# Fused attention and feed-forward kernel: the last tokens of each head projected on quarter tiles, and the weight product in one piece between the projections

## The chip, the cores and the metric

One core of one Trainium2 chip. The metric is the device time of one execution in microseconds, lower is better. Before the change, the median of three runs is 926.65 us (926.5 to 930.34).

## The reference

```python
def phi(x):                                  # x: (4, 8, 576, 64), w_phi: (64, 128)
    proj = np.einsum('bhsd,df->bhsf', x, w_phi)
    proj = proj - np.max(np.abs(proj), axis=-1, keepdims=True)
    return np.concatenate([np.exp(proj), np.exp(-proj)], axis=-1)
q_p, k_p = phi(q), phi(k)
kv = np.einsum('bhsf,bhsd->bhfd', k_p, v)
z = np.sum(k_p, axis=2)
num = np.einsum('bhsf,bhfd->bhsd', q_p, kv)
den = np.einsum('bhsf,bhf->bhs', q_p, z)[..., None] + 1e-06
x = (num / den) -> (2304 tokens, 512)
h = ((x @ w1) * (x @ w2)) @ w3               # w1, w2: 512x1024, w3: 1024x1024
x = h @ w_out                                # 1024x512
r = np.maximum(x @ w_in, 0.0)                # 512x2048
out = (r * r) @ w_out2                       # 2048x512
```

All arrays are float32.

## The kernel before

The kernel has two stages on one core. The first is attention over 16 pairs of heads, to about 253 us of the span. It also makes the product w3 @ w_out, so that the first feed-forward needs one matrix where the reference has two. The second stage is both feed-forwards; the change doesn't touch it.

Each engine has its instruction stream written out by hand, and the streams meet on semaphores; nothing reorders them. A pair is two heads of 576 tokens, one in partitions 0 to 63 (h0), the other in 64 to 127 (h1), features by tokens. 576 tokens are four chunks of 128 and a tail of 64. One pair on TensorE, in order:

1. `first_half`: wait for k's load, for the previous zq and for the previous tail exponential; project k (`project`, L459 the chunks, L461 the tail) into `ps_proj`; the numerators of the previous pair's first half of tokens (L482, with 64-column tiles, and L490, the denominators with 32-column tiles); a quarter of a weight product (L551, six matmuls); wait for q and for zk; project q; the numerators of the second half of tokens.
2. `second_half`: `kv_sign(0)` (L466, L468), another quarter of the weight product, wait for zq, `transpose_features` (L474, L475), `kv_sign(1)`.

The quarters of the weight product run from pair 3 on: 24 matmuls for each of eight 128-row pieces of w3, of which pairs 3 to 15 do two quarters each; the last three halves come after the pairs. In a projection the tokens are the stationary operand. Each chunk is a 64-row matmul, alternating between the row halves; the tail is one 128-row matmul over both heads, whose operand is padded: the two heads' tails stand in separate columns with zeros in the other head's rows, so q and k have 640 columns instead of 576, and phi is stored in three blocks. A float32 matmul is two load and two matmul instructions in the trace.

DVE, per pair: after the k projection a reduction to the largest absolute value (L588) and an addition (L593) give zk; then a piece of the previous output (L280); the same for q gives zq; then the low halves of the weight product (L610) and of the next w3 piece (L86); the inverse of the denominators (L272, L274). ACT: copies of numerators (L667), exponentials of zk (L660), the high halves of the weight product (L693) and of w3 (L80), exponentials of the transposed zq (L648 for the tail, L652), a copy of kv (L673). SyncE issues all transfers in one hand-written order; the loads of q, k and v for a pair go out about one pair ahead. DVE and ACT split the first unit of feed-forward weights behind pair 3 as well (L186, L180).

Of the kernel before, what the change touches and what calls it, by code (L numbers as in the profile page):

```python
# [23 lines left out]
P = 128  # L24
BATCH, HEADS, SEQ, HEAD_DIM, FEAT = 4, 8, 576, 64, 128
PAIRS = BATCH * HEADS // 2
# [2 lines left out]
CHUNKS = SEQ // P  # L29
TAIL = SEQ - CHUNKS * P  # L30
FULL = CHUNKS * P
WIDE = FULL + 2 * TAIL
SLOTS = 2 * CHUNKS + 1
VW = HEAD_DIM + 1

# [253 lines left out]
def attention(nc, ins, ident_dram, x_dram, d_dram, r_dram, wprod, raw, ff):  # L289
    qT, kT, v_full, v_tail, w_phi, wout_dram, w3_dram, wu_dram = ins  # L290
    with ExitStack() as ctx:  # L291
        def sb(name, shape, dt=F32):
            return ctx.enter_context(nc.sbuf_tensor(name, shape, dt))
# [6 lines left out]

        ident = sb("ident", [P, P])

        phi_raw = sb("phi_raw", [P, 3, FEAT])
        q_raw = [sb(f"q_raw{s}", [P, WIDE]) for s in range(2)]
        k_raw = [sb(f"k_raw{s}", [P, WIDE]) for s in range(2)]
        vs = [sb(f"vs{s}", [P, CHUNKS + 1, 2, VW]) for s in range(2)]
        neg_max_k = sb("neg_max_k", [P, SLOTS])
        neg_max_q = sb("neg_max_q", [P, SLOTS])
# [46 lines left out]
        @block.sync  # L355
        def _(sp):
            def load_qkv(n, s, reused):

                if reused:
                    sp.wait_ge(kproj_done, n - 1)  # L360
                sp.dma_start(k_raw[s][:, :], kT[n]).then_inc(k_loaded[s], 16)
                if reused:
                    sp.wait_ge(qproj_done, n - 1)
                sp.dma_start(q_raw[s][:, :], qT[n]).then_inc(q_loaded[s], 16)
                if reused:
                    sp.wait_ge(kv_done, n - 1)
                load_v(n, s)

            def load_v(n, s):
                for h in range(2):  # L370
                    sp.dma_start(vs[s][:, 0:CHUNKS, h, 0:HEAD_DIM], v_full[n, :, :, h]).then_inc(v_loaded[s], 16)
                sp.dma_start(vs[s][:, CHUNKS, :, 0:HEAD_DIM], v_tail[n]).then_inc(v_loaded[s], 16)

            sp.dma_start(k_raw[0][:, :], kT[0]).then_inc(k_loaded[0], 16)
            sp.dma_start(phi_raw[:, :, :], w_phi).then_inc(phi_loaded, 16)
            sp.dma_start(q_raw[0][:, :], qT[0]).then_inc(q_loaded[0], 16)
            sp.dma_start(ident[:, :], ident_dram).then_inc(ident_loaded, 16)

            sp.wait_ge(v_framed, 2)
            load_v(0, 0)  # L380
            load_qkv(1, 1, False)
            for i in range(2):
                sp.dma_start(raw.slots[i][:, :], wout_dram[i]).then_inc(raw.loaded[i], 16)

            def load_piece(slot, src, pieces):

                sp.wait_ge(raw.lo, pieces)
                sp.dma_start(raw.slots[slot][:, :], src).then_inc(raw.loaded[slot], 16)

            def results(n, s):  # L390

                store_den(sp, ff, n - 1, 1 - s, 1, d_dram)
                load_den(sp, ff, n - 1, d_dram)
                spread_rden(sp, ff, n - 1, r_dram)

            for i in range(2, WOUT_CHUNKS):
                load_piece(i % 2, wout_dram[i], i - 1)
            store_den(sp, ff, 0, 0, 0, d_dram)
            load_qkv(2, 0, True)
            results(1, 1)  # L400
            load_piece(0, w3_dram[0], WOUT_CHUNKS - 1)
            sp.wait_ge(raw.lo, WOUT_CHUNKS)
            load_unit(sp, ff, wu_dram, 0)
            store_den(sp, ff, 1, 1, 0, d_dram)
            load_qkv(3, 1, True)
            store_x(sp, ff, 0, x_dram)
            results(2, 0)
            store_den(sp, ff, 2, 0, 0, d_dram)
            load_qkv(4, 0, True)
            load_piece(0, w3_dram[1], PIECE_W3 + 1)  # L410
            store_x(sp, ff, 1, x_dram)
            results(3, 1)


            with sp.Fori(2, PAIRS // 2 - 1) as i:
                store_den(sp, ff, 2 * i - 1, 1, 0, d_dram)
                load_qkv(2 * i + 1, 1, True)
                store_x(sp, ff, 2 * i - 2, x_dram)
                results(2 * i, 0)
                store_den(sp, ff, 2 * i, 0, 0, d_dram)  # L420
                load_piece(0, w3_dram[i], PIECE_W3 + i)
                load_qkv(2 * i + 2, 0, True)
                store_x(sp, ff, 2 * i - 1, x_dram)
                results(2 * i + 1, 1)
            store_den(sp, ff, PAIRS - 3, 1, 0, d_dram)
            load_qkv(PAIRS - 1, 1, True)
            store_x(sp, ff, PAIRS - 4, x_dram)
            results(PAIRS - 2, 0)
            store_den(sp, ff, PAIRS - 2, 0, 0, d_dram)
            load_piece(0, w3_dram[KF1 - 1], PIECE_W3 + KF1 - 1)  # L430
            load_x(sp, ff, x_dram, 0)
            store_x(sp, ff, PAIRS - 3, x_dram)
            results(PAIRS - 1, 1)
            sp.wait_ge(raw.lo, PIECE_W3 + KF1)
            load_unit(sp, ff, wu_dram, 1)
            store_den(sp, ff, PAIRS - 1, 1, 0, d_dram)
            store_x(sp, ff, PAIRS - 2, x_dram)
            store_den(sp, ff, PAIRS - 1, 1, 1, d_dram)
            load_den(sp, ff, PAIRS - 1, d_dram)
# [13 lines left out]
        def _(pe):  # L453
            def project(src):

                for c in range(CHUNKS):
                    for h in range(2):
                        rows = slice(h * HEAD_DIM, (h + 1) * HEAD_DIM)
                        pe.matmul(ps_proj[:, CHUNKS * h + c, :], src[rows, c * P:(c + 1) * P], phi_raw[rows, h, :],  # L459
                                  start=(c == 0), stop=True, skip_group_check=True)  # L460
                return pe.matmul(ps_proj[:, 2 * CHUNKS, :], src[:, FULL:WIDE], phi_raw[:, 2, :], start=True, stop=True)  # L461

            def kv_sign(sign, s):
                for h in range(2):
# [31 lines left out]
            def first_half(n, s, turn, w=None):  # L496


                pe.wait_ge(k_loaded[s], 16 * (turn + 1))
                pe.wait_ge(zq_done, n)  # L500
                pe.wait_ge(eq_tail_done, n)
                project(k_raw[s]).then_inc(kproj_done, 1)
                if previous(n):
                    first_numerators(n - 1)
                if w:
                    w_product(*w)

                pe.wait_ge(q_loaded[s], 16 * (turn + 1))
                pe.wait_ge(zk_done, n + 1)
                project(q_raw[s]).then_inc(qproj_done, 1)  # L510
                if previous(n):
                    last_numerators(n - 1)
# [8 lines left out]
                pe.wait_ge(ff.num_copied, 2 * n + 1)  # L521
                numerators(1).then_inc(numB_done, 1)

            def second_half(n, s, turn, w=None):

                pe.wait_ge(v_loaded[s], 48 * (turn + 1))
                pe.wait_ge(ek_done, 2 * n + 1)

                pe.wait_ge(kv_copied, n)
                kv_sign(0, s)  # L530
                if w:
                    w_product(*w)

                pe.wait_ge(zq_done, n + 1)
                pe.wait_ge(eq_done, n)
                transpose_features().then_inc(t_done, 1)
                pe.wait_ge(ek_done, 2 * n + 2)
                kv_sign(1, s).then_inc(kv_done, 1)

            def w_product(m, part, parts=4):  # L540

                if part == 0:

                    pe.wait_ge(raw.hi, m + PIECE_W3 + 1)
                    pe.wait_ge(wp_lo, m)
                steps = [(i, a, b, k) for i, (a, b) in enumerate(TERMS) for k in range(KF1)]
                n = len(steps) // parts
                for i, a, b, k in steps[part * n:(part + 1) * n]:
                    if a == LO and k == 0:
                        pe.wait_ge(raw.lo, m + PIECE_W3 + 1)  # L550
                    last = pe.matmul(ps_w[:, :], w3[:, a, k * P:(k + 1) * P],  # L551
                                     wout[:, b, k * D_MODEL:(k + 1) * D_MODEL],
                                     start=(i == 0 and k == 0), stop=(i == 2 and k == KF1 - 1))
                if part == parts - 1:
                    last.then_inc(wp_done, 1)

            pe.wait_ge(phi_loaded, 16)
# [6 lines left out]
            first_half(2, 0, 1)  # L564
            second_half(2, 0, 1)
            first_half(3, 1, 1, (0, 0))
            second_half(3, 1, 1, (0, 1))
            with pe.Fori(2, PAIRS // 2) as i:
                first_half(2 * i, 0, i, (i - 2, 2))
                second_half(2 * i, 0, i, (i - 2, 3))  # L570
                first_half(2 * i + 1, 1, i, (i - 1, 0))
                second_half(2 * i + 1, 1, i, (i - 1, 1))

            w_product(KF1 - 2, 1, 2)
            first_numerators(PAIRS - 1)
            w_product(KF1 - 1, 0, 2)
            last_numerators(PAIRS - 1)
            w_product(KF1 - 1, 1, 2)


        @block.vector
# [612 lines left out]
```

## Time and profile before

| | before |
|---|---|
| median of three runs | 926.65 us |
| lowest, highest | 926.5, 930.34 us |
| profiled execution, its own time | 926.82 us |
| its span | 925.0 us |
| TensorE matmul, load | 900.7 us (97%), 796.7 us (86%) |
| DVE, ACT, GpSimd | 584.9 us (63%), 409.3 us (44%), 219.4 us (24%) |
| mean granted TensorE clock | 0.998 of full speed |

Busy times are shares of the span. PE is TensorE's matmul side, PEld its weight loads, which run beside matmuls. In an operand shape such as 64\*128 the first number is the rows that a tile of the array uses and the second its columns. The ends of matmuls are modelled and overlap the next ones, so it is starts that should be compared.

### The profile page before, as it was taken

To read this page: it belongs to the slowest core of one execution; us is meant where nothing else is said; L and a number is where in the kernel's file an instruction comes from. 1 tells how busy PE (TensorE), PEld (TensorE's weight loads), DVE (VectorE), ACT (ScalarE), POOL (GpSimd) and SP (SyncE) were. 2 spreads that over 40 slices of the span, in tenths; PEclk is the share of its full clock that TensorE was granted. 3 is DMA by queue.
4 is the path that set the end of the run, shared out by engine and by line. 5 is a ranking of instruction groups with operands and counts; after the bars stand their busy time and mean duration, and the time that the engine had idled before them with its cause. 6 is when DMAs were issued, how large, how long until landed. Compare 5 with 4: busy or idle time off the path is not lost. (4 is left out here: it accounts for less than half of the span.)

```text
span 925.0 us, 15179 instructions
## 1 busy us (share of the span) xinstructions
PE 900.7 (97%) x5712; PEld 796.7 (86%) x5712; DVE 584.9 (63%) x732; ACT 409.3 (44%) x675; POOL 219.4 (24%) x222
## 2 busy tenths in 40 slices
PE   6889999999989999999999999999999999999998
PEld 6768787777679999999999998989889888989897
DVE  3554545454467666666666678776777776666652
ACT  3534543444443445344534464444544344634433
POOL 0100000000336324432353216322143222213100
PEclk9999999999999999999999999999999999999999
DMA  6544345352441112311331232321133212132201
GB/s 188 158 117 138 100 129 147 109 154 83 153 162 35 52 44 102 115 46 46 114 114 46 69 136 86 121 90 48 62 144 114 92 46 91 46 119 87 69 23 69
DMA packets 62023, 89.32 MB, mean 97 GB/s; under 512 B 29840, under 2 KB 40464, under 8 KB 61200
## 3 DMA queue, kind: packets, MB, share of 16 engines
q1 hardware_dynamic: 61968, 88.58, 29.3%
q8 instruction: 35, 0.57, 0.3%
q14 instruction: 20, 0.16, 0.1%
HBM read 74.26 MB, written 14.30 MB: 96 GB/s over the span
## 5 line engine op out<-in xcount | busy, mean ns | idle before, releaser
L851 PE MATMUL banks<-xc,wc 128*128 128x384 f32 x2016 | 411.3, 339 | 7.7 <-PEq L291 3.5
L851 PEld LDWEIGHTS banks<-xc,wc 128*128 128x128 f32 x2016 | 360.2, 189 | 31.5 <-issue 6.6
L931 ACT COPY s<-banks 128x384 f32<-128x384 f32 x144 | 69.1, 480 | 236.7 <-PE banks L851 236.7
L155 POOL TENSOR_TENSOR w_raw<-w_raw 128x256 f32<-128x256 f32 x48 | 37.3, 778 | 442.5 <-DMA w_raw<-in_w_units 442.5
L1042 DVE TENSOR_TENSOR c<-s,banks 128x384 f32<-128x384 f32 x144 | 79.5, 552 | 95.1 <-PE banks L851 60.7
L186 DVE TENSOR_TENSOR wc<-w_raw,wc 128x1024 fp32r<-128x1024 f32 x96 | 117.9, 1236 | 23.9 <-ACT wc L180 23.9
L1051 DVE TENSOR_TENSOR pg<-c,pg 128x384 fp32r<-128x384 f32 x120 | 93.9, 788 | 44.2 <-ACT pg L938 43.4
L895 PE MATMUL banks<-wprod_hi,pg 128*128 128x512 f32 x432 | 113.0, 393 | 0.0
L895 PE MATMUL banks<-wprod_lo,pg 128*128 128x512 f32 x432 | 112.2, 393 | 0.0
L938 ACT CAST pg<-c 128x384 fp32r<-128x384 f32 x120 | 61.9, 515 | 93.9 <-DVE c L1099 55.4
L873 PE MATMUL banks<-pg,wprod_hi 128*128 128x256 f32 (+1 forms) x384 | 97.8, 338 | 1.0 <-DVE pg L1051 1.0
L895 PEld LDWEIGHTS banks<-wprod_lo,pg 128*128 128x128 f32 x432 | 80.0, 188 | 12.2
L180 ACT CAST wc<-w_raw 128x1024 fp32r<-128x1024 f32 x96 | 90.5, 945 | 0.0
L895 PEld LDWEIGHTS banks<-wprod_hi,pg 128*128 128x128 f32 x432 | 80.0, 188 | 11.9
L873 PEld LDWEIGHTS banks<-pg,wprod_hi 128*128 128x128 f32 x384 | 68.0, 188 | 1.9 <-DVE pg L1051 1.9
L873 PE MATMUL banks<-pg,wprod_lo 128*128 128x512 f32 x192 | 65.2, 340 | 0.0
L466 PEld LDWEIGHTS ps_kv<-vs,ek 128*128 128x128 f32 x512 | 61.3, 196 | 3.4 <-issue 3.4
L466 PE MATMUL ps_kv<-vs,ek 128*128 128x65 f32 x512 | 63.9, 279 | 0.0
L201 POOL TENSOR_TENSOR x_sum<-x_raw 128x768 f32<-128x768 f32 x6 | 12.4, 2065 | 193.5 <-DMA x_raw<-x_raw_dram 193.5
L551 PE MATMUL ps_w<-wout,w 128*128 128x512 f32 x192 | 51.9, 408 | 0.0
L160 POOL TENSOR_TENSOR w_raw<-w_raw 128x256 f32<-128x256 f32 x48 | 48.9, 1020 | 0.0
L1046 DVE SCALAR_TENSOR_TENSOR c<-c 128x384 f32<-128x384 f32 x72 | 46.9, 652 | 2.5
(68 smaller groups left out, 930.5 us busy)
## 6 DMA issues: line engine op xcount, KB each, us to landing
w_raw<-in_w_units SPq DMA_DIRECT2D x48, 384.0 KB, 3.9
wo_raw<-in_w_out SPq DMA_DIRECT2D x24, 512.0 KB, 3.5
w_raw<-in_w_units SPq DMA_DIRECT2D x48, 128.0 KB, 3.9
k_raw<-in_kT SPq DMA_DIRECT2D x16, 320.0 KB, 3.0
q_raw<-in_qT SPq DMA_DIRECT2D x16, 320.0 KB, 3.9
stage<-r_dram SPq DMA_DIRECT2D x32, 144.0 KB, 3.0
x_raw_dram<-stage SPq DMA_DIRECT2D x16, 288.0 KB, 3.5
x_raw<-x_raw_dram SPq DMA_DIRECT2D x3, 1536.0 KB, 6.6
```

What stands on the lines that cost most here:

```text
L160: pool.tensor_tensor(s4, a12, s2, ALU.subtract).then_inc(ff.s4_made, 1)
L180: act.copy(hi, raw).then_inc(ff.wc_hi, 1)
L186: dve.tensor_tensor(lo, raw, hi.bitcast(F32), ALU.subtract).then_inc(ff.wc_lo, 1)
L466: pe.matmul(ps_kv_v[:, sign, h, :], ek[:, sign, CHUNKS * h + c, :], vs[s][:, c, h, :], start=(c == 0 and h == 0 and sign == 0), stop=False ...
L551: last = pe.matmul(ps_w[:, :], w3[:, a, k * P:(k + 1) * P], wout[:, b, k * D_MODEL:(k + 1) * D_MODEL], start=(i == 0 and k == 0), stop=(i ...
L851: last = pe.matmul(bank, ff.wc[u % 2][:, w, i, k * P:(k + 1) * P], x[:, a, k, :], start=(i in (P1, P2, P5) and t == 0 and k == 0), stop=(t ...
L873: last = pe.matmul(acc[b][:, cols], wprod[w][:, j * D_MODEL + n * P:j * D_MODEL + (n + 1) * P], pg[u % 2][:, a, 0, tokens], start=(j == 0 ...
L895: last = pe.matmul(acc[c], pg[u % 2][:, a, f, c * P:(c + 1) * P], wo[u % 2][:, w, f * D_MODEL:(f + 1) * D_MODEL], start=(j == 0 and m == 0 ...
L931: act.copy(out[:, :], y_bank).then_inc(copied, 1)
L938: act.copy(pg[u % 2][:, HI, f, half * TB:(half + 1) * TB], raw[:, :]).then_inc(pg_hi, 1)
L1042: dve.tensor_tensor(out[:, :], {P2: s1, P5: s3, P3: s2}[i][:, :], z_bank, ALU.add).then_inc(done, 1)
L1051: dve.tensor_tensor(pg[u % 2][:, LO, f, cols], raw[:, :], pg[u % 2][:, HI, f, cols].bitcast(F32), ALU.subtract).then_inc(pg_lo, 1)
```

## The change

The tail of each head becomes a matmul of its own, with 64 rows and 64 stationary columns (64 tokens), in the head's row half and with its output in the head's partition half. The order is h0 chunk 0, h1 tail, h0 chunk 1, h1 chunk 0, h0 chunk 2, h1 chunk 1, h0 chunk 3, h1 chunk 2, h0 tail, h1 chunk 3. The weight product runs in halves of twelve matmuls, all between the two projections, and none in `second_half`. q and k lose their padding (576 columns), phi is 128 by 128 and is the first transfer.

```diff
-        phi_raw = sb("phi_raw", [P, 3, FEAT])
-        q_raw = [sb(f"q_raw{s}", [P, WIDE]) for s in range(2)]
-        k_raw = [sb(f"k_raw{s}", [P, WIDE]) for s in range(2)]
+        phi_raw = sb("phi_raw", [P, FEAT])
+        q_raw = [sb(f"q_raw{s}", [P, SEQ]) for s in range(2)]
+        k_raw = [sb(f"k_raw{s}", [P, SEQ]) for s in range(2)]
...
+            sp.dma_start(phi_raw[:, :], w_phi).then_inc(phi_loaded, 16)
             sp.dma_start(k_raw[0][:, :], kT[0]).then_inc(k_loaded[0], 16)
-            sp.dma_start(phi_raw[:, :, :], w_phi).then_inc(phi_loaded, 16)
             sp.dma_start(q_raw[0][:, :], qT[0]).then_inc(q_loaded[0], 16)
...
             def project(src):
 
-                for c in range(CHUNKS):
-                    for h in range(2):
-                        rows = slice(h * HEAD_DIM, (h + 1) * HEAD_DIM)
-                        pe.matmul(ps_proj[:, CHUNKS * h + c, :], src[rows, c * P:(c + 1) * P], phi_raw[rows, h, :],
-                                  start=(c == 0), stop=True, skip_group_check=True)
-                return pe.matmul(ps_proj[:, 2 * CHUNKS, :], src[:, FULL:WIDE], phi_raw[:, 2, :], start=True, stop=True)
+
+                def chunk(h, c):
+                    rows = slice(h * HEAD_DIM, (h + 1) * HEAD_DIM)
+                    if c < CHUNKS:
+                        return pe.matmul(ps_proj[:, CHUNKS * h + c, :], src[rows, c * P:(c + 1) * P],
+                                         phi_raw[rows, :], start=(c == 0), stop=True, skip_group_check=True)
+                    return pe.matmul(ps_proj[rows, 2 * CHUNKS, :], src[rows, FULL:SEQ], phi_raw[rows, :],
+                                     start=True, stop=True, skip_group_check=True)
+
+                for c in range(CHUNKS + 1):
+                    chunk(0, c)
+                    last = chunk(1, (c - 1) % (CHUNKS + 1))
+                return last
...
-            def second_half(n, s, turn, w=None):
+            def second_half(n, s, turn):
...
                 kv_sign(0, s)
-                if w:
-                    w_product(*w)
...
-            def w_product(m, part, parts=4):
+            def w_product(m, part):
...
-                n = len(steps) // parts
+                n = len(steps) // 2
...
             first_half(3, 1, 1, (0, 0))
-            second_half(3, 1, 1, (0, 1))
+            second_half(3, 1, 1)
             with pe.Fori(2, PAIRS // 2) as i:
-                first_half(2 * i, 0, i, (i - 2, 2))
-                second_half(2 * i, 0, i, (i - 2, 3))
+                first_half(2 * i, 0, i, (i - 2, 1))
+                second_half(2 * i, 0, i)
                 first_half(2 * i + 1, 1, i, (i - 1, 0))
-                second_half(2 * i + 1, 1, i, (i - 1, 1))
```

The rest of the diff drops the host's padding of q, k and phi and adapts the three calls of `w_product` behind the loop, which do the same as before.

## Rows read from the trace of the kernel before

**Rows 1.** The page: busy time of the engines; the chain by engine.

```profile
PE 900.7 (97%) x5712; PEld 796.7 (86%) x5712; DVE 584.9 (63%) x732; ACT 409.3 (44%) x675; POOL 219.4 (24%) x222
...
PE 48%; DVE 1%; ACT 0%; issue 0%; ACTq 0%
```

**Rows 2.** Windows, one pair: busy time (instructions) by engine, granted clock, DMA.

```profile
152.41:167.11 14.70, 14.70 (x143) 11.52 (x142) 8.12 (x8) 6.69 (x12) 0.00 (x0) 1.00 0.37 108
```

**Rows 3.** Waits up to 300 us: total us, times, longest.

```profile
PE ps_proj L459 <- DVE zk L593: 8.3, 5, 2.9
```

**Rows 4.** TensorE in order of time: start, us from first start to last end.

```profile
152.41 1.16 PE L459 MATMUL ps_proj<-phi_raw,k_raw 64*128 64x128 f32 x16
153.50 0.49 PE L461 MATMUL ps_proj<-phi_raw,k_raw 128*128 128x128 f32 x2
153.92 1.19 PE L482 MATMUL ps_num<-eq,kv 128*64 128x288 f32 x8
155.04 0.70 PE L490 MATMUL ps_num<-eq,kv 128*32 128x144 f32 x16
155.67 1.66 PE L551 MATMUL ps_w<-wout,w 128*128 128x512 f32 x6
157.26 1.16 PE L459 MATMUL ps_proj<-phi_raw,q_raw 64*128 64x128 f32 x16
...
162.35 0.44 PE L468 MATMUL ps_kv<-vs,ek 128*128 128x130 f32 x2
162.54 1.64 PE L551 MATMUL ps_w<-wout,w 128*128 128x512 f32 x6
164.02 1.04 PE L474 MATMUL ps_t<-ident,zq 128*128 128x128 f32 x8
```

**Rows 5.** Weight loads in order of time, the same pair.

```profile
152.41 0.97 PEld L459 LDWEIGHTS ps_proj<-phi_raw,k_raw 64*128 64x128 f32 x16
...
155.04 0.40 PEld L490 LDWEIGHTS ps_num<-eq,kv 128*32 128x32 f32 x16 [0.44 <-issue]
```

**Rows 6.** Instructions of lines 459 and 482: duration in ns, least, median, most.

```profile
L459 PEld LDWEIGHTS ps_proj<-phi_raw,k_raw x256: 182/188/330, 4.3 to 226.7; 64*128 64x128 f32 x128
L459 PE MATMUL ps_proj<-phi_raw,k_raw x256: 271/272/578, 4.3 to 226.8; 64*128 64x128 f32 x128
...
L482 PEld LDWEIGHTS ps_num<-eq,kv x152: 132/137/138, 100.0 to 232.8; 128*64 128x64 f32 x152
```

**Rows 7.** In order of time: the first projection, and DVE behind the second pair's.

```profile
4.25 2.08 PE L459 MATMUL ps_proj<-phi_raw,k_raw 64*128 64x128 f32 x16 [4.25 <-DMA phi_raw<-in_w_phi]
...
6.26 0.79 PE L461 MATMUL ps_proj<-phi_raw,k_raw 128*128 128x128 f32 x2
...
21.99 1.36 DVE L588 TENSOR_REDUCE neg_max_k<-ps_proj 128x9 f32<-128x1152 f32 x1 [4.14 <-PE ps_proj L461]
```

**Rows 8.** Windows, the first 20 us.

```profile
0.00:20.00 20.00, 12.81 (x79) 12.10 (x80) 7.95 (x12) 7.12 (x9) 1.42 (x6) 1.00 0.67 195
```

**Rows 9.** TensorE in order of time, pair 2.

```profile
29.98 0.44 PE L468 MATMUL ps_kv<-vs,ek 128*128 128x130 f32 x2
30.26 1.04 PE L474 MATMUL ps_t<-ident,zq 128*128 128x128 f32 x8
```

**Rows 10.** TensorE in order of time, behind the last pair.

```profile
240.41 2.98 PE L551 MATMUL ps_w<-wout,w 128*128 128x512 f32 x12
```

**Rows 11.** In order of time: DVE in pair 3, TensorE in pairs 3 and 4.

```profile
48.74 1.16 DVE L86 TENSOR_TENSOR w<-w_raw,w 128x1024 fp32r<-128x1024 f32 x1
...
52.71 1.16 PE L459 MATMUL ps_proj<-phi_raw,q_raw 64*128 64x128 f32 x16 [1.41 <-DVE zk L593]
...
69.08 1.16 PE L459 MATMUL ps_proj<-phi_raw,q_raw 64*128 64x128 f32 x16 [1.61 <-DVE zk L593]
```

**Rows 12.** DVE in order of time, the pair of rows 4.

```profile
160.27 1.36 DVE L593 TENSOR_TENSOR zq<-ps_proj,neg_max_q 128x1152 f32<-128x1152 f32 x1
```

**Rows 13.** Transfers: KB each, median us from issue to landing.

```profile
k_raw<-in_kT SPq DMA_DIRECT2D x16, 320.0 KB, 3.0
```

More of the change, by code:

```diff
@@ L31 @@
 FULL = CHUNKS * P
-WIDE = FULL + 2 * TAIL
 SLOTS = 2 * CHUNKS + 1
@@ L553, in w_product @@
                                      start=(i == 0 and k == 0), stop=(i == 2 and k == KF1 - 1))
-                if part == parts - 1:
+                if part == 1:
                     last.then_inc(wp_done, 1)
@@ L566, in _ @@
             first_half(3, 1, 1, (0, 0))
-            second_half(3, 1, 1, (0, 1))
+            second_half(3, 1, 1)
             with pe.Fori(2, PAIRS // 2) as i:
-                first_half(2 * i, 0, i, (i - 2, 2))
-                second_half(2 * i, 0, i, (i - 2, 3))
+                first_half(2 * i, 0, i, (i - 2, 1))
+                second_half(2 * i, 0, i)
                 first_half(2 * i + 1, 1, i, (i - 1, 0))
-                second_half(2 * i + 1, 1, i, (i - 1, 1))
-            w_product(KF1 - 2, 1, 2)
+                second_half(2 * i + 1, 1, i)
+            w_product(KF1 - 2, 1)
             first_numerators(PAIRS - 1)
-            w_product(KF1 - 1, 0, 2)
+            w_product(KF1 - 1, 0)
             last_numerators(PAIRS - 1)
-            w_product(KF1 - 1, 1, 2)
+            w_product(KF1 - 1, 1)
         @block.vector
@@ L1145, in stacked @@
     def stacked(a):
-        t = a.transpose(0, 1, 3, 2).reshape(PAIRS, 2, HEAD_DIM, SEQ)
-        wide = np.zeros((PAIRS, 2, HEAD_DIM, WIDE), a.dtype)
-        wide[..., :FULL] = t[..., :FULL]
-        for h in range(2):
-            wide[:, h, :, FULL + h * TAIL:FULL + (h + 1) * TAIL] = t[:, h, :, FULL:]
-        return wide.reshape(PAIRS, P, WIDE)
+        return pack(a.transpose(0, 1, 3, 2).reshape(PAIRS, P, SEQ))
     qT, kT = stacked(q), stacked(k)
@@ L1160 @@
     v_tail = v_tail.reshape(PAIRS, P, 2, HEAD_DIM)
-    phi_blocks = np.zeros((P, 3, FEAT), w_phi.dtype)
-    for h in range(2):
-        rows = slice(h * HEAD_DIM, (h + 1) * HEAD_DIM)
-        phi_blocks[rows, h] = w_phi
-        phi_blocks[rows, 2] = w_phi
+    phi_twice = pack(np.concatenate([w_phi, w_phi]))
     w3 = pack(moe_w3.T.reshape(KF1, P, KF1, P).transpose(2, 1, 0, 3).reshape(KF1, P, W_CHUNK))
@@ L1185 @@
     arrays = {
-        "qT": qT, "kT": kT, "v_full": v_full, "v_tail": v_tail, "w_phi": phi_blocks, "w3": w3, "w_out": w_out,
+        "qT": qT, "kT": kT, "v_full": v_full, "v_tail": v_tail, "w_phi": phi_twice, "w3": w3, "w_out": w_out,
         "w_units": w_units, "w_out2": w_out2, "identity": np.eye(P, dtype=np.float32),
```

## The prediction

> **What bounds the kernel now.** I read the page first. TensorE is busy for 97% of the span, and the chain that ended last stays on it [rows 1], so the question is what the change does to TensorE's queue, not to DVE, ACT or the transfers. Every line of the diff belongs to attention, which ends near 253 us. The windows show what a pair is there: 14.70 us, TensorE busy for all of it, and two more pairs in a row take the same [rows 2]. So in the steady part, what TensorE's instructions take is what the pair takes. There are 16 pairs.
>
> The waits name the exceptions [rows 3]: in attention five waits of a projection of q for the shifted k (zk), one in each of pairs 0 to 4, 8.3 us together.
>
> The view in order of time then shows how one group of matmuls follows another [rows 4]. Ends are modelled, so I set each start against the modelled end before it. Where the shape stays 128\*128, the next group starts 0.16 to 0.25 us before that end: 162.54 against 162.35 + 0.44 = 162.79, 164.02 against 164.18. Where the shape changes it is always 0.07: 153.50 against 152.41 + 1.16 = 153.57 (64\*128 to 128\*128), 153.92 against 153.99 (to 128\*64), 155.04 against 155.11 (to 128\*32), 155.67 against 155.74 (to 128\*128), 157.26 against 157.33 (to 64\*128). After a change the first load starts with the first matmul, and the load side had sat idle 0.44 us before 155.04 [rows 5]. So a change of tile shape empties the pipe and then exposes the first load. The change to 128\*32 tells most: its first tile (columns 0 to 31) shares no column with the last one before it (64 to 127), and it waits all the same.
>
> The Trainium skill has this as a rule (TensorEngine Tiling (Array Packing), Key Properties): changing the tiling mode, not just the tile, drains TensorE. The five changes above agree with it. It lists 64×128 and 64×64 as two configurations; no row of this trace has a 64\*64 tile.
>
> **The change, part by part.**
>
> *Tail on quarter tiles.* A projection is now 16 half-array instructions, 153.50 − 152.41 = 1.09 us, and 2 full ones, 153.92 − 153.50 = 0.42: 1.51 us [rows 4]. After the change it is 20: a 64\*128 chunk (2), the h1 tail 64\*64 (2), six 64\*128 chunks (12), the h0 tail (2), a chunk (2). Four changes of shape inside are new, and the one to the full tail goes. The trace doesn't show a 64\*64 tile, so I bound it.
>
> - All four cost what every change here costs: then a lone matmul of two instructions is like the full tail, load exposed, second load behind it, drain: 0.42 us. A tail loads 64 columns, 0.137 us against 0.188 [rows 6]: 0.37. The run of twelve is that of sixteen less four steps; a step is (0.97 − 0.19)/15 = 0.052 by loads [rows 5], (1.16 − 0.27)/15 = 0.059 by matmuls [rows 4, 6]; with 0.055, 1.09 − 0.22 = 0.87. Sum 0.42 + 0.37 + 0.87 + 0.37 + 0.42 = 2.45, +0.94. The full tail is the nearest row (as many instructions, as wide an operand, a change on both sides), and I take this value.
> - Cheapest drain: only a longer step. The last half matmul started at 152.41 + 1.16 − 0.27 = 153.30, the next group at 153.50: 0.20 for 0.055. A lone matmul: (0.49 − 0.27)/2 = 0.11, and 0.20, 0.31; the twelve 11 × 0.059 + 0.20 = 0.85. Sum 2.09, +0.58.
> - Dearest: 4 × 0.42 + 0.85 = 2.53, +1.02.
> - No drain: 1.09 + 4 × 0.055 = 1.31, −0.20.
>
> *Where it counts.* In pairs 5 to 15 TensorE never waits, so both projections count. In pairs 0 to 2 the wait for zk runs from the end of the projection of k, for which DVE had been idle (4.14 us in pair 1 [rows 7]): both count too. In the first pair instructions take about twice as long (16 in 6.26 − 4.25 = 2.01 us, the tail 0.79 − 0.07 = 0.72), at a granted clock of 1.00 [rows 7, 8]: 2 × 0.72 + 2 × 0.62 + 2.01 − 4 × 0.12 = 4.21 against 2.73, +1.48. Pairs 3 and 4 are below. So 2 × 1.48 + 13 × 2 × 0.94 = 27.4 us.
>
> *Weight product in one piece.* Its 192 instructions stay; in pairs 3 to 15 the six behind kv_sign(0) move between the projections. Taken away: last kv group to transposes 164.02 − 162.35 = 1.67 us [rows 4], 30.26 − 29.98 = 0.28 in a pair without them [rows 9]: 1.39. Added: twelve before a change of shape take 2.98 − 0.07 = 2.91 [rows 10], six 157.26 − 155.67 = 1.59 [rows 4]: 1.32. Eleven pairs × −0.07 = −0.8; with 0.2 of doubt at an end, −3 to +1.5.
>
> *Pairs 3 and 4.* Here the six more cover a wait of the q projection for zk, 1.41 and 1.61 us. zk was late because DVE was in a split (48.74 + 1.16 = 49.90 in pair 3) when the k projection had long ended [rows 11]. That split hangs on the pair before, so a k projection 0.94 later is swallowed too. q then starts later by 0.94 + 1.32 − 1.41 = 0.85 and 0.65 us; with the q projection +0.94 and the six gone −1.39 that is +0.4 and +0.2, +0.6 together. With no drain q starts when zk lets it, as now, and each pair gives −0.20 − 1.39 = −1.59.
>
> *What the six covered behind kv_sign(0).* The transposes could start at 162.35 + 0.28 = 162.63 [rows 4, 9]; zq is done at 160.27 + 1.36 = 161.63 [rows 12]: 1.0 us to spare. ACT's and DVE's halves of the product come earlier, ahead of the exponentials of q instead of among them. The next k projection needs the tail exponential, the numerators the copy of kv; both move with the transposes or ahead, and TensorE waited for neither: nothing gained. SyncE's next w3 piece waits for DVE's half, now earlier.
>
> *Unpadded q and k, smaller phi, phi first.* 288 KB for 320 a load; a load of k lands in 3.0 us [rows 13] and is issued almost a pair ahead: hidden. At the start TensorE waits until 4.25 us for phi [rows 7], issued second; now k is second. With 3.0 us to land for k too it is 0, between −0.5 and +0.3.
>
> **Sum.** Against the profiled execution, 926.82 us (span 925.0; 0.2 above the runs' median): 926.8 + 27.4 − 0.8 + 0.6 = 954 us, +2.9%. Its own ends: cheapest 926.8 + 14 × 1.16 − 0.8 (pairs 3 and 4) − 0.8 = 941; dearest 926.8 + 13 × 2.04 + 3.4 + 0.9 + 1.5 = 959.
>
> **Rivals.**
> *No drain (the other side).* The 64\*64 tiles flow within their row halves. For it: the halves overlap here, a step of 0.055 against 0.11 alone. Against: none of the five changes of shape escaped. It decides at each projection's second matmul: a start 0.05 after the first, not 0.4. 926.8 − 13 × 0.40 − 2 × 0.24 − 2 × 1.59 − 0.8 = 917 us.
> *Waiting within a row half only*, where a tail and a chunk follow each other in it: two waits of 0.15 (0.20 − 0.055), 1.31 + 0.30 = 1.61, +0.10. 14 × 0.20 + 2 × (0.10 − 1.39) − 0.8 = −0.6: 926 us. Against: the change to 128\*32, as above.
> *The transposes wait for zq*, from the point at which it is 1.0 us later; at most 1.39 × 13 = 18 us: with no drain, up to 935. Pair 2 has that order already, and its transposes follow the last kv group by only 0.28 [rows 9].
>
> **How the numbers follow.** Drain 0.70, no drain 0.17, within a half 0.11, zq 0.02. One measurement of this kernel tells 0.5% (4.6 us) from no change. Slower 0.70 + 0.02, same 0.11, faster 0.17. The likeliest alone: 941 to 959. The range takes in the within-a-half case and 4 us below it, and leaves out most of no drain: 921 to 960.
>
> **What would show it.** Right: matmuls of shape 64\*64 on TensorE, 64 each for k and q; a projection of about 2.45 us in order of time, each change of shape 0.07 before the modelled end; the load side idle inside it; a pair of 16.5 us; no wait for zk in pairs 3 and 4; everything behind attention shifted and otherwise alike. Wrong: 20 instructions in 1.3 us and a pair of 14.2; or a gap before the transposes put down to zq.

## The result, and the profile after

The changed kernel takes 956.07 us (median of four runs, 955.01 to 962.57); the kernel before, run on the same chip, 928.5 (926.5 to 930.61). The ratio on record is 1.031, 95% interval 1.026 to 1.037 (it is estimated from the runs, and is not exactly the quotient of the two medians, 1.030). The prediction was 954 us. The profiled execution after took 955.01 us, its span is 953.2, that is 28.2 more than before. One run of all that are told of here, 963.53 us in e6, stands as slow beside the others of its kernel, and its ratio leaves it out.

The page: TensorE's busy time has risen from 900.7 us [rows 1] by 32.1 us. That is 3.9 more than the span, because TensorE also waits less: 3.0 us for zk, 0.7 at the start of the feed-forward and 0.2 for the first load. DVE, ACT and GpSimd do what they did.

```profile
PE 932.8 (98%) x5776; PEld 812.9 (85%) x5776; DVE 584.5 (61%) x732; ACT 409.2 (43%) x675; POOL 220.9 (23%) x222
...
PE 47%; DVE 1%; ACT 0%; issue 0%; ACTq 0%
```

One steady pair in windows (busy time and instructions by engine, granted clock), to be read against [rows 2]: 16.47 us in place of 14.70, still with no idle TensorE, at a clock of 1.00 in both.

```profile
154.06:170.53 16.47, 16.47 (x146) 12.46 (x145) 6.49 (x7) 5.80 (x10) 0.00 (x0) 1.00 0.42 124
```

TensorE in order of time, the same stretch of a pair as [rows 4]. The lines that answer to them are the projections: what was two rows is five.

```profile
154.06 0.48 PE L459 MATMUL ps_proj<-phi_raw,k_raw 64*128 64x128 f32 x2
154.48 0.43 PE L461 MATMUL ps_proj<-phi_raw,k_raw 64*64 64x128 f32 x2
154.84 0.94 PE L459 MATMUL ps_proj<-phi_raw,k_raw 64*128 64x128 f32 x12
155.70 0.43 PE L461 MATMUL ps_proj<-phi_raw,k_raw 64*64 64x128 f32 x2
156.06 0.48 PE L459 MATMUL ps_proj<-phi_raw,k_raw 64*128 64x128 f32 x2
156.48 1.19 PE L488 MATMUL ps_num<-eq,kv 128*64 128x288 f32 x8
...
158.23 3.01 PE L555 MATMUL ps_w<-wout,w 128*128 128x512 f32 x12
161.17 0.49 PE L459 MATMUL ps_proj<-phi_raw,q_raw 64*128 64x128 f32 x2
...
167.17 0.44 PE L474 MATMUL ps_kv<-vs,ek 128*128 128x130 f32 x2
167.45 1.04 PE L480 MATMUL ps_t<-ident,zq 128*128 128x128 f32 x8
```

From start to start: 0.42 + 0.36 + 0.86 + 0.36 + 0.42 = 2.42 us a projection, where it was 1.51. And after each change of shape the next group starts 0.06 to 0.08 us before the modelled end in front of it, also where the next matmul works in the other half of the rows: 154.48 against 154.06 + 0.48 = 154.54, 154.84 against 154.91. The transposes follow the last kv group by 0.28, as in [rows 9].

The load side of the q projection says the same. Load and matmul start together at each change (the matmul groups of this projection start at 161.17, 161.58, 161.94, 162.81 and 163.17 us), and before a wide load the load side sits idle (last column):

```profile
161.58 0.19 PEld L461 LDWEIGHTS ps_proj<-phi_raw,q_raw 64*64 64x64 f32 x2
161.94 0.75 PEld L459 LDWEIGHTS ps_proj<-phi_raw,q_raw 64*128 64x128 f32 x12 [0.17 <-issue]
162.81 0.19 PEld L461 LDWEIGHTS ps_proj<-phi_raw,q_raw 64*64 64x64 f32 x2
163.17 0.29 PEld L459 LDWEIGHTS ps_proj<-phi_raw,q_raw 64*128 64x128 f32 x2 [0.17 <-issue]
```

The waits of TensorE over the whole span, against [rows 3]: the wait for zk is left in three pairs of five.

```profile
PE ps_proj L459 <- DVE zk L597: 5.3, 3, 2.9
PE ps_proj L459 <- DMA k_raw<-in_kT: 4.1, 1, 4.1
```

Cut at the start of k projections, the two traces add up like this (us; forecast is the term of the prediction's sum):

| stretch | before | after | change | forecast |
|---|---|---|---|---|
| to the first matmul | 4.25 | 4.06 | −0.2 | 0 |
| pair 0 | 16.13 | 20.11 | +4.0 | +3.0 |
| pairs 1 and 2 | 26.00 | 31.05 | +5.1 | +3.8 |
| pair 3 | 16.17 | 16.47 | +0.3 | +0.4 |
| pair 4 | 16.38 | 16.48 | +0.1 | +0.2 |
| pairs 5 to 14 | 146.96 | 164.73 | +17.8 | +18.1 |
| pair 15 to the first feed-forward matmul | 30.48 | 31.53 | +1.1 | +1.8 |
| feed-forward | 668.6 | 668.8 | +0.1 | 0 |

### The profile page after: what moved, and what is told of

Same layout as the page of the kernel before. It is cut to its first block and busy times, and to the rows that moved or that the text cites. A ratio compares the mean times of both kernels' runs of the same rounds, so it can differ in the third digit from the quotient of the medians.

```text
span 953.2 us, 15307 instructions
## 1 busy us (share of the span) xinstructions
PE 932.8 (98%) x5776; PEld 812.9 (85%) x5776; DVE 584.5 (61%) x732; ACT 409.2 (43%) x675; POOL 220.9 (23%) x222
## 5 line engine op out<-in xcount | busy, mean ns | idle before, releaser
L154 POOL TENSOR_TENSOR w_raw<-w_raw 128x256 f32<-128x256 f32 x48 | 37.3, 778 | 447.2 <-DMA w_raw<-in_w_units 447.2
L671 ACT COPY stage<-ps_num 128x432 f32<-128x432 f32 x32 | 16.6, 520 | 110.6 <-PE ps_num L496 110.6
L592 DVE TENSOR_REDUCE neg_max_q<-ps_proj 128x9 f32<-128x1152 f32 x16 | 21.7, 1359 | 54.0 <-PE ps_proj L459 54.0
L592 DVE TENSOR_REDUCE neg_max_k<-ps_proj 128x9 f32<-128x1152 f32 x16 | 21.7, 1359 | 50.8 <-PE ps_proj L459 50.8
```

What stands on the lines that cost most here:

```text
L154: pool.tensor_tensor(s1, a21, a22, ALU.add).then_inc(ff.s1_made, 1)
L592: dve.tensor_reduce(neg_max[:, :], ps_proj[:, 0:SLOTS, :], AX.X, ALU.max, negate=True, apply_absolute_value=True).then_inc(m_done, 1)
```

## The experiments

Times are medians beside the kernel before on the same chip (927.4 us in all three sets); the ratio is to that kernel, with its 95% interval. e1 to e4 ran on one chip, e5 and e6 on a second, e8 and e9 on a third, so between these sets it is the ratios that should be compared. Diffs are cut to the lines that matter, against the changed kernel unless said otherwise. "Projection" and "pair" are start to start in the steady part of each profile.

**e1, tails last.** One change of shape inside a projection instead of four.

```diff
-                for c in range(CHUNKS + 1):
-                    chunk(0, c)
-                    last = chunk(1, (c - 1) % (CHUNKS + 1))
+                for c in (0, 1, 2, 3, 4):
+                    for h in range(2):
+                        last = chunk(h, c)
```

> The changed kernel with only the order in a projection altered: eight 64*128 chunks, then both 64*64 tails next to each other. One change of shape inside the projection instead of four. If each change of shape empties the pipe (my theory), the tails' four instructions cost one exposed load of 64 columns, overlapping streams and one drain, about 0.43 us, and a projection is 1.09 + 0.43 = 1.52 us instead of 2.42; a steady pair is 16.48 - 1.80 = 14.68 us and the kernel 923 to 925 us. Rival 1, the quarter tile itself is slow (0.36 us for each tail wherever it stands): the projection is 1.09 + 0.72 = 1.81, a pair 15.3, the kernel 933. Rival 2, only a change within one row half makes the array wait: here each half has one such change, half as many as now, so some half of the 1.1 us over free flow remains: 1.85 us, 933.

Measured: 924.62 us, ratio 0.996 (0.993 to 0.999). TensorE in order of time:

```profile
152.29 1.16 PE L459 MATMUL ps_proj<-phi_raw,k_raw 64*128 64x128 f32 x16
153.38 0.44 PE L461 MATMUL ps_proj<-phi_raw,k_raw 64*64 64x128 f32 x4
153.74 1.19 PE L488 MATMUL ps_num<-eq,kv 128*64 128x288 f32 x8
```

Four instructions on quarter tiles take 0.36 us here, as long as two of them do when they stand alone. So the quarter tile is not slow (rival 1 falls), 1.45 us is also far from the 1.85 of rival 2, and one change inside costs nothing over before: projection 1.45 us, pair 14.56. The order alone is worth about 31 us, 956 against 925. The tails were somewhat cheaper than the 0.43 that I expected. No run has both tails in front of the chunks.

**e2, tails in the middle.** The order (0, 1, 4, 2, 3): two changes inside.

> As e1, but both tails stand behind the second round of chunks: two changes of shape inside the projection. By the count of changes: 0.65 + 0.43 + 0.65 = 1.73 us a projection, a steady pair 15.1 us, the kernel about 931 us. If the quarter tile itself were slow, moving it would change nothing against e1. The steps from e1 (one change inside) to e2 (two) to the changed kernel (four) give the price of one change: about 0.21 from one to two, and 0.7 for the next two with the lone matmuls that then lose their overlap with the other row half.

Measured: 930.05 us, ratio 1.002 (0.999 to 1.005).

```profile
152.56 0.71 PE L459 MATMUL ps_proj<-phi_raw,k_raw 64*128 64x128 f32 x8
153.20 0.44 PE L461 MATMUL ps_proj<-phi_raw,k_raw 64*64 64x128 f32 x4
153.57 0.71 PE L459 MATMUL ps_proj<-phi_raw,k_raw 64*128 64x128 f32 x8
154.21 1.19 PE L488 MATMUL ps_num<-eq,kv 128*64 128x288 f32 x8
```

0.64 + 0.37 + 0.64 = 1.65 us: the same twenty instructions as e1, one more change, +0.20. The groups of 8, 12 and 16 take 0.64, 0.86 and 1.09: about 0.21 us a group and 0.055 an instruction. From two changes to four the price is 0.77 and not 0.40, since the four groups of two also lose their partner in the other half (0.42 against 0.21 + 0.11).

**e3, quarter tails alone.** The weight product back in quarters.

```diff
-                first_half(2 * i, 0, i, (i - 2, 1))
-                second_half(2 * i, 0, i)
+                first_half(2 * i, 0, i, (i - 2, 2))
+                second_half(2 * i, 0, i, (i - 2, 3))
...
```

> The changed kernel with the weight product back in quarters: the quarter tails and the transfers alone. By my sum the quarter tiles carry the whole loss: projections 2.42 us, steady pair 14.70 + 1.82 = 16.52 us, and in pairs 3 and 4 the waits for zk stay, so these take 17.1 and 17.3 instead of 16.5 us: 957 us, about 2 over the changed kernel. If instead the moved weight product cost something, this would be faster than the changed kernel's 956.

Measured: 955.26 us, ratio 1.029 (1.023 to 1.034); profiled span 953.8 against 953.2. Projection 2.42, pair 16.5, pairs 3 and 4 16.5 and 17.3 us. The tails carry the whole loss. The 2 us that the moved product should save beside them do not show in the medians; in the profile only pair 4 differs clearly (17.3 against 16.5), pair 3 had 16.5 and not the 17.1 that I expected.

**e4, one piece alone.** The tail is one full-array matmul again.

```diff
-                    return pe.matmul(ps_proj[rows, 2 * CHUNKS, :], src[rows, FULL:SEQ], phi_raw[rows, :],
-                                     start=True, stop=True, skip_group_check=True)
...
+                return pe.matmul(ps_proj[:, 2 * CHUNKS, :], src[:, FULL:WIDE], phi_raw[:, :], start=True, stop=True)
```

> The changed kernel with the tail back as one full-array matmul over padded operands; the weight product stays in one piece, phi is small and first. By my sum: projection 1.51 us, steady pair 14.65, pairs 3 and 4 each 1.4 us shorter than before since the waits for zk (1.41 and 1.61 us) are covered by the six more matmuls, first matmul 0.2 us earlier: 926.8 - 2.8 - 0.6 - 0.2 = 923 us, 0.4% below before. Rival, that nothing is gained because the cover only moves to the wait for zq: then a gap before the transposes shows and the time is 927 or more.

Measured: 924.34 us, ratio 0.996 (0.993 to 0.998). Pair 14.66, as expected; pair 3 has come down from 16.17 to 14.91 us, but pair 4 only from 16.38 to 15.96. e1 differs from this kernel only in the tail and its padding; its pair is 0.10 us shorter, and the medians (924.62 and 924.34) show no gain. In order of time, pair 4:

```profile
57.25 0.55 SPq L246 DMA_DIRECT2D d_dram<-stage  x1
...
62.38 0.32 SPq L253 DMA_DIRECT2D stage<-d_dram  x1
64.08 0.17 DVE L272 TENSOR_SCALAR stage<-stage 128x9 f32<-128x9 f32 x1 [5.97 <-DMA stage<-d_dram]
64.29 0.21 DVE L274 RECIPROCAL stage<-stage 128x9 f32<-128x9 f32 x1
64.42 2.03 DVE L186 TENSOR_TENSOR wc<-w_raw,wc 128x1024 fp32r<-128x1024 f32 x2
69.27 1.16 PE L460 MATMUL ps_proj<-phi_raw,q_raw 64*128 64x128 f32 x16 [1.23 <-DVE zk L592]
```

The denominators leave for memory at 57.25 and are back at 64.08, 6.8 us later. DVE stands at their inversion for 5.97 us and only then splits the weights and makes zk. That trip did not get shorter with the pair: before it took 5.9 us (56.65 to 62.57), in e5 7.1 (55.90 to 63.00), where e5's next one took 3.5 (72.25 to 75.75). What stretches it in pair 3 is not shown. So zk is late in pair 4, and TensorE waits 1.23 us in spite of six more matmuls as cover.

**e5, one shape.** The order of the changed kernel, but the tails are 64\*128 matmuls over padded operands, summed into one output. Both write the same bank from different halves, so a semaphore orders them.

```diff
-                    return pe.matmul(ps_proj[rows, 2 * CHUNKS, :], src[rows, FULL:SEQ], phi_raw[rows, :],
-                                     start=True, stop=True, skip_group_check=True)
+                    if h == 0:
+                        pe.wait_ge(tail_h1, count)
+                    m = pe.matmul(ps_proj[:, 2 * CHUNKS, :], src[rows, FULL:WIDE], phi_raw[rows, :],
+                                  start=(h == 1), stop=True, skip_group_check=True)
+                    return m.then_inc(tail_h1, 1) if h == 1 else m
...
```

> The changed kernel's own order, but no 64*64 tile: each tail is a 64*128 matmul over a 128-column operand padded with zeros (tail and zeros for h0, zeros and tail for h1), both summed into the same output, the second ordered behind the first by a semaphore. More columns loaded and no change of shape inside the projection. By my theory nothing drains: 1.09 + 4 * 0.055 = 1.31 us a projection (up to 0.1 more for the semaphore), steady pair 14.25 to 14.4 us, and 10 to 12 us less than e1's sum at four changes: kernel 918 to 920, below before. Rival, a tail alone in the middle of chunks is what costs, whatever its shape: projection near 2.42, pair 16.5, 956.

Measured: 918.89 us, ratio 0.991 (0.988 to 0.994): faster than both kernels. Line 461 is the chunks, line 465 the tails; the first rows are h0's chunk and h1's tail, which start together.

```profile
147.90 0.37 PE L461 MATMUL ps_proj<-phi_raw,k_raw 64*128 64x128 f32 x1
147.90 0.37 PE L465 MATMUL ps_proj<-phi_raw,k_raw 64*128 64x128 f32 x1
148.11 0.27 PE L461 MATMUL ps_proj<-phi_raw,k_raw 64*128 64x128 f32 x1
148.12 0.27 PE L465 MATMUL ps_proj<-phi_raw,k_raw 64*128 64x128 f32 x1
148.22 0.84 PE L461 MATMUL ps_proj<-phi_raw,k_raw 64*128 64x128 f32 x12
...
149.21 1.19 PE L493 MATMUL ps_num<-eq,kv 128*64 128x288 f32 x8
```

Twenty instructions in 149.21 − 147.90 = 1.31 us, with a tail still second and ninth. More columns are loaded than in the changed kernel, and it is 1.11 us faster a projection: it is the shape that costs, not the place of a tail, and the semaphore costs nothing that can be seen (0.21 + 20 × 0.055 = 1.31).

**e6, halves in turn.** As e1 (against which this diff is), but all chunks of h0 and then all of h1, to price lost overlap without more changes of shape.

```diff
-                for c in (0, 1, 2, 3, 4):
-                    for h in range(2):
-                        last = chunk(h, c)
+                for h in range(2):
+                    for c in range(CHUNKS):
+                        chunk(h, c)
+                for h in range(2):
+                    last = chunk(h, CHUNKS)
```

> As e1 (tails last, one change of shape inside), but all chunks of h0 and then all of h1, so that no two row halves overlap. It prices the second half of what a lone matmul loses. With 0.107 us a step instead of 0.055 the sixteen take 0.11 + 16 * 0.107 + 0.10 = 1.92 us instead of 1.09, the tails stay at 0.36: projection 2.28, steady pair 14.56 + 1.66 = 16.2 us, kernel about 950. If the loss in the changed kernel were all from draining and none from lost overlap, this would stay near e1's 925.

Measured: 941.22 us, ratio 1.014 (1.011 to 1.017), where I had said 950. Three of its runs took 939.93 to 941.51 us, one 963.53.

```profile
152.00 1.71 PE L459 MATMUL ps_proj<-phi_raw,q_raw 64*128 64x128 f32 x16
153.64 0.43 PE L461 MATMUL ps_proj<-phi_raw,q_raw 64*64 64x128 f32 x4
154.01 1.19 PE L490 MATMUL ps_num<-eq,kv 128*64 128x288 f32 x8
```

Sixteen take 1.64 us in place of 1.09; a step within one half is (1.71 − 0.27)/15 = 0.096 us, not 0.107, and the whole group is 0.28 shorter than the 1.92 expected; twice that in each of 16 pairs is the 9 us by which I missed. Lost overlap is a real price, 0.04 us an instruction, but the smaller one: eight lone instructions of it in the changed kernel are, as an estimate, 0.3 of the 1.1 us.

**e8, split earlier.** e5 (against which this diff is), with the split of the first weight unit moved into pair 3, ahead of the inversion; the same on ACT.

```diff
+                if unit:
+                    w_lo(dve, ff, 0, 0)
+                    w_lo(dve, ff, 0, 1)
                 if previous(n):
                     invert_den(dve, ff, n - 1)
...
```

> e5 with one more edit: ACT's and DVE's split of the first unit of feed-forward weights (lines 180 and 186 in e5's trace) moves from behind pair 3 into it, behind zq, ahead of the inversion of the denominators. In e4 and e5 pair 4 kept a wait for zk of 1.2 and more, since DVE stands at the inversion until the denominators have gone through memory (63.00 us in e5) and only then does the split (2.03 us) and zk. If that queue on DVE is the cause, the wait for zk in pair 4 falls from about 1.7 to under 0.2 us, pair 4 from 16.03 to about 14.5, and the kernel is about 1.5 us below e5, 917. If the cause were the numerators or ACT, the wait would stay.

Measured: 919.7 us, ratio 0.991 (0.988 to 0.994), so no gain over e5 that can be measured, where I had expected 917 us. In the profile pair 4 does what was expected; in windows, e5 and then e8 (first busy time is TensorE's):

```profile
60.42:76.45 16.03, 14.36 (x146) 11.41 (x145) 10.74 (x13) 8.89 (x14) 0.00 (x0) 1.00 0.36 105
```

```profile
60.12:74.41 14.29, 14.29 (x146) 11.41 (x146) 8.88 (x11) 7.23 (x12) 0.00 (x0) 1.00 0.40 114
```

The wait is gone and pair 4 is 1.74 us shorter, as expected. But the trip of the denominators was shorter here as well, 5.6 us (55.60 to 61.18) against 7.1. As an estimate from e5's rows, a trip 1.5 us shorter would have brought zk from 68.14 to about 66.6, and that alone would have left some 0.1 to 0.2 of the 1.67 us of waiting. So the wait came of the trip and of DVE's order behind it together, and e8 doesn't show what the order alone is worth.

**e9, one shape with quarters.** e5 with the weight product in quarters, as in the kernel before.

> e5 with the weight product back in quarters: one shape within the projection alone. Projections 1.31 us, steady pair 14.70 - 0.40 = 14.30 us, pairs 3 and 4 keep their waits for zk (1.4 and 1.6 us or a little more): about 1.5 to 2.5 us over e5, 921. If the piece moved is worth nothing, it equals e5.

Measured: 922.31 us, ratio 0.994 (0.991 to 0.997). Against e5 (0.988 to 0.994) the intervals touch; the medians say 3.4 us for the piece moved, and e4 is 3.1 below before, with an interval that lies below 1; but there phi's change is in it, and e3 beside after shows no gain. So some 3 us for the piece moved are suggested and not shown by themselves. Its pairs 3 and 4 took 15.32 and 16.17 us, e5's 14.28 and 16.03.

| kernel | changes inside | projection | steady pair | ratio |
|---|---|---|---|---|
| before | 1 (full tail) | 1.51 | 14.70 | 1 |
| e4, one piece alone | 1 (full tail) | 1.51 | 14.66 | 0.996 |
| e5, one shape | 0 | 1.31 | 14.29 | 0.991 |
| e1, tails last | 1 | 1.45 | 14.56 | 0.996 |
| e2, tails in the middle | 2 | 1.65 | 14.99 | 1.002 |
| after | 4 | 2.42 | 16.47 | 1.031 |

All of these but before have the weight product in one piece and phi small and first, so the ratios should be read beside e4's.

## Why the prediction was right

**The tail on quarter tiles.** Forecast 2.45 us a projection, measured 2.42: lone chunks 0.42 and 0.42, tails 0.36 for 0.37, the twelve 0.86 for 0.87. The full tail of [rows 4] was the right nearest row, and the bounds of 2.09 and 2.53 held. It is shown by e1, e2 and e5 that the changes of shape set most of this: the same projection takes 1.31, 1.45, 1.65 and 2.42 us with none, one, two and four. Some 0.3 us of the last is the overlap with the other half that lone matmuls lose (e6); the forecast had it inside its 0.42 for a lone matmul. The drain doesn't look at which rows are in use: a tail in the other half waited in full, so the rival "within a row half" falls on the rows of after, and "no drain" with it. The time that was worked out for it, 917 us, is about what e5 takes, the kernel in which nothing changes shape (918.89). The Trainium skill's rule (TensorEngine Tiling (Array Packing), Key Properties), that a change of tiling mode drains TensorE, holds here for 64×128 against 64×64 as well; the runs price it at 0.21 us a group.

**Where it counts.** Pairs 5 to 14 gave 17.8 us for a forecast of 18.1. Pairs 0 to 2 gave 2.3 us more than forecast, and it is not the projections that did. In pair 0 these gave +3.1 (from k's first matmul to q's first 7.23 us for 5.74, q's projection 4.22 for 2.60), as forecast. The other 0.9 lies behind them: TensorE's instructions take twice as long up to about 22.7 us of the span (in the group at 21.44, 2.53 us, they change over), where before that ended at about 18.1. Where this ends is chance as far as the runs show: at about 19.4 us in e5 and 13.5 in e9, whose instructions are the same up to there. And in pair 2 a stretch of 4.1 us had a granted clock of 0.58 in the mean, so most of it stood at the lower of the two levels (1.2 GHz of 2.4). The rows after, windows first, then the order of time:

```profile
46.00:50.10 4.10, 4.10 (x31) 1.89 (x29) 2.72 (x2) 0.46 (x1) 1.86 (x3) 0.58 1.10 344
```

```profile
46.78 2.19 PE L488 MATMUL ps_num<-eq,kv 128*64 128x288 f32 x8
48.90 1.19 PE L496 MATMUL ps_num<-eq,kv 128*32 128x144 f32 x16
```

These two groups take 3.24 us there and 1.75 in the steady pairs, so 1.5 us. TensorE had waited 1.19 us for zk in that pair before it. e3, with the same projections, has such a stretch too (0.91 in the window from 20 to 40 us), while the other eight profiles have none before 240 us. Whether the longer projections bring it about stays open; these are two profiles, and no run was made for it. Such stretches also come and go within one kernel: in its 55 runs beside the experiments the kernel before had mean clocks between 0.993 and 1.000 and took 922.01 to 934.76 us. So these 2.3 us are no part of what was forecast, and it is luck that other terms came out 1.3 us lower together.

**The weight product.** Twelve take 161.17 − 158.23 = 2.94 us before a change, so 1.35 more than six (forecast 1.32), against the 1.39 taken away: nothing, as said. The transposes had no wait for zq, so that rival falls too.

**Pairs 3 and 4.** +0.3 and +0.1 against +0.4 and +0.2: the waits for zk are gone. That the late k projection would be swallowed was right. The part of it that is wrong concerns the rival: with no drain q was to start "when zk lets it, as now". But counted from the start of pair 4 zk let it start later than before, by 1.0 us in e4 and 1.2 in e5, because the denominators' trip through memory doesn't shrink with the pair; in pair 3 of e5 it could start 0.3 earlier. Each of these pairs was to be worth −1.59 us; e5 has 14.28 − 16.17 = −1.89 and 16.03 − 16.38 = −0.35.

**Transfers.** The first matmul starts 0.19 us earlier, now behind k's load; forecast 0 with −0.5 to +0.3. Nothing else of it shows. Behind attention the feed-forward is shifted and alike; the wait at its start is 2.8 us against 3.5, which gives 0.7 back, unforecast.

## What to carry to other kernels

Count changes of tile shape in TensorE's stream as instructions of their own: a smaller tile for a leftover loses where it stands alone among another shape. Put next to each other, the quarter tiles here were no faster in the medians than the full-array tail (e1 beside e4); what paid was to pad the leftover to the shape around it (e5). In a trace, compare each start with the modelled end before it; where the lead over it falls to one small fixed value (here 0.07 us), the pipe was emptied, and the nearest such group prices the next one to within some hundredths. A transfer round trip in the middle of an engine's queue can become the next wait when the work around it shrinks.

## What was not expected of the hardware

Two quarter-tile matmuls in opposite row halves, one behind the other, take 0.36 us together (e1), as long as one alone (after). In e5 the matmuls of both halves start within 0.01 us of each other in the steady pairs, while two matmuls in one half step by 0.096 us (e6), less than the 0.107 that the second load of a lone matmul suggested.
